# An attention stage woven into a matmul stage: other slots for the pieces from the fourteenth pair on, and another order of four small steps

## The reference

```python
# attention in chunks of 64 rows, per batch and head: q, k, v (8, 8, 576, 64)
scores = scale * q_c @ k_c.T ; scores -= max(scores) ; attn = exp(scores)
attn = attn / (sum(attn) + 1e-9) ; out = attn @ v_c
x = out as (4608, 512)
# first feed-forward, d_ff 1536
xn = x / sqrt(mean(x * x) + 1e-6) * rms_g
y = (silu(xn @ w_gate) * (xn @ w_val)) @ w_out
# second feed-forward, d_ff 2048
h = y @ w_in2 ; g = h * clip(h + 3, 0, 6) / 6 ; result = g @ w_out2
```

## Time and profile before

| | |
|---|---|
| median of 3 runs | 1655.23 us (1655.1 to 1658.37) |
| profiled execution, time | 1649.52 us |
| profiled execution, span | 1647.7 us |
| mean granted TensorE clock | 0.995 |
| PE busy | 1612.2 us (98%) |
| DVE, ACT, POOL busy | 1054.4, 859.0, 786.0 us |
| attention woven in | from about 45 us to about 357 us |

### The profile page before, as it was taken

How to read it: one execution, slowest core, us unless ns; L and a number is a source line. 1 busy time by engine, 2 the same in 40 slices (tenths; PEclk the granted TensorE clock), 3 DMA queues, 4 the chain that set the end, 5 groups by cost and what they waited for, 6 DMA issues and landing times.

```text
span 1647.7 us, 29730 instructions
## 1 busy us (share of the span) xinstructions
PE 1612.2 (98%) x11337; PEld 1572.1 (95%) x11337; DVE 1054.4 (64%) x1441; ACT 859.0 (52%) x1341; POOL 786.0 (48%) x772
## 2 busy tenths in 40 slices
PE   7889999999999999999999999999999999999998
PEld 5778898899999999999999999999999999999998
DVE  5877878868755555665555776656666865455454
ACT  4756666655544445554444565555655644434432
POOL 2543443449776665434240477777676631231231
PEclk9999999999999999999999999999999999999999
DMA  9677776644565655989997866556658986776674
GB/s 180 141 190 157 171 196 167 156 149 141 190 223 196 209 196 197 337 312 314 310 315 283 301 235 237 207 190 239 225 192 268 390 273 202 219 230 211 211 227 118
DMA packets 335646, 366.88 MB, mean 223 GB/s; under 512 B 186256, under 2 KB 299152, under 8 KB 332304
## 3 DMA queue, kind: packets, MB, share of 16 engines
q1 hardware_dynamic: 321584, 334.69, 64.1%
q0 software_dynamic: 8800, 28.85, 5.1%
q10 hardware_dynamic: 5120, 1.44, 0.5%
HBM read 200.80 MB, written 164.10 MB: 221 GB/s over the span
## 4 chain that ended last, share of the span: by engine, by line
PE 87%; DVE 3%; POOL 3%; issue 2%; SPq 2%; ACT 2%; DMA 1%; DVEq 0%; ACTq 0%; POOLq 0%
PE bx L968 14%; PE by L968 14%; PE bx L970 14%; PE bx L969 14%; PE by L970 14%; PE by L969 14%; SPq L568 1%; PE att L946 1%; DVE tx L1498 1%; PE att L895 1%; PE att L937 1%; DMA hl_b<-h_scratch 1%; PE att L918 1%; DVE wr L1511 1%; SPq L561 0%
## 5 line engine op out<-in xcount | busy, mean ns | idle before, releaser
L968 PE MATMUL bx<-tx,wr 128*128 128x384 f32 x840 | 288.0, 343 | 4.1 <-ACT gb L1176 2.0
L968 PE MATMUL by<-tx,wr 128*128 128x384 f32 x840 | 287.2, 342 | 0.1
L970 PE MATMUL bx<-tx,wr 128*128 128x384 f32 x840 | 281.9, 336 | 0.0
L969 PE MATMUL bx<-tx,wr 128*128 128x384 f32 x840 | 281.6, 335 | 0.0
L970 PE MATMUL by<-tx,wr 128*128 128x384 f32 x840 | 281.5, 335 | 0.0
L969 PE MATMUL by<-tx,wr 128*128 128x384 f32 x840 | 281.4, 335 | 0.0
L1549 DVE TENSOR_TENSOR hl_d<-hl_d 128x1536 fp32r<-128x1536 f32 x84 | 146.6, 1775 | 91.2 <-ACT hl_d L1248 91.2
L1867 POOL DMA_DIRECT2D out_dram<-ot x128 | 70.2, 556 | 248.3 <-DVE ot L1572 245.8
L1549 DVE TENSOR_TENSOR hl_b<-hl_b 128x1152 fp32r<-128x1152 f32 x84 | 117.9, 1419 | 105.5 <-ACT hl_b L1248 104.6
L1248 ACT ACTIVATE hl_d<-hl_d 128x1536 fp32r<-128x1536 f32 x84 | 123.3, 1486 | 112.5 <-DMA hl_d<-u_scratch 112.5
L968 PEld LDWEIGHTS bx<-tx,wr 128*128 128x128 f32 x840 | 158.2, 188 | 9.3 <-issue 3.1
(11 more groups left out here) (193 smaller groups left out, 3781.4 us busy)
## 6 DMA issues: line engine op xcount, KB each, us to landing
hl_d<-u_scratch SPq DMA_DIRECT2D x84, 768.0 KB, 4.5
hl_b<-h_scratch SPq DMA_DIRECT2D x84, 576.0 KB, 5.5
u_scratch<-ut SPq DMA_DIRECT2D x48, 576.0 KB, 3.7
h_scratch<-ht SPq DMA_DIRECT2D x36, 576.0 KB, 3.7
u_scratch<-ub SPq DMA_DIRECT2D x96, 192.0 KB, 2.8
u_scratch<-ub SPq DMA_DIRECT2D x48, 384.0 KB, 2.5
h_scratch<-vb SPq DMA_DIRECT2D x72, 192.0 KB, 3.3
h_scratch<-vb SPq DMA_DIRECT2D x36, 384.0 KB, 3.0
```

What stands on the lines that cost most here:

```text
L968: pe.matmul(dst, w_hi, m_hi, start=start, stop=False, skip_group_check=not opens)
L969: pe.matmul(dst, w_hi, m_lo, start=False, stop=False, skip_group_check=not opens)
L970: return pe.matmul(dst, w_lo, m_hi, start=False, stop=stop, skip_group_check=not opens)
```

## The change

For the pairs from 13 on, the slots of the four pieces are written anew. From pair 17 on AT of a pair lies in the slot of SC of the next pair (it was one slot behind it), and TensorE does AT first. XX lies five slots behind AT as before, and so in the slot of TR of the next pair, behind it. The pairs 13 to 17 lead over to that pattern. `AFTER` has new entries for when q and k of the next pair are transposed. The order of four steps within a slot changes too: ScalarE copies the probabilities ahead of the snapshots and of the mean square; VectorE scales the attention ahead of the maxima; GpSimd's inverse root comes at AT+2 in place of AT+3.

```diff
-    EARLY = {... 13: (38, 43, 48, 51), 14: (46, 49, 52, 58), 15: (51, 53, 59, 64), 16: (57, 61, 66, 73), 17: (64, 66, 75, 77)}
-    AFTER = {7: 5, 8: 1, 11: 5, 12: 5, 14: 1, 16: 5, 17: 5}
+    EARLY = {... 13: (40, 43, 46, 50), 14: (45, 49, 52, 57), 15: (51, 56, 59, 63), 16: (58, 62, 64, 68), 17: (63, 68, 70, 76)}
+    AFTER = {7: 5, 8: 1, 11: 5, 12: 5, 25: 5, 20: 1, 24: 1, 33: 1, 29: 5, 30: 1, 15: 5, 17: 3, 18: 3, 23: 5, 32: 5, 28: 3, 13: 3, 26: 3, 16: 3, 22: 1, 34: 1, 19: 5, 21: 5, 27: 3}
...
-        return EARLY[n][piece] if n in EARLY else 7 * n - 53 - min(3, (n - 12) // 2) + (0, 5, 8, 13)[piece]
+        return EARLY[n][piece] if n in EARLY else 7 * n - 53 - min(3, (n - 12) // 2) + (0, 5, 7, 12)[piece]
...  ScalarE, in each slot
+                n = woven(m, slot, TR, 1)
+                if n is not None:
+                    copy_probsT(n)
                 if slot in (1, 2):
                     snap_a(m, S1, slot - 1)
...
                 n = woven(m, slot, AT, 2)
                 if n is not None:
                     mean_square(n)
-                n = woven(m, slot, TR, 1)
-                if n is not None:
-                    copy_probsT(n)
...  VectorE, in each slot
+                n = woven(m, slot, AT, 1)
+                if n is not None:
+                    scale_attention(n)
                 n = woven(m, slot, SC, 1)
                 if n is not None and n + 1 < NN and next_transposed_after(n) == 1:
                     transpose_qk(n + 1)
                 if n is not None:
                     shift_scores(n)
-                n = woven(m, slot, AT, 1)
-                if n is not None:
-                    scale_attention(n)
...  GpSimd, in each slot
-                n = woven(m, slot, AT, 3)
+                n = woven(m, slot, AT, 2)
                 if n is not None:
                     inverse_rms(n)
```

More of the change, by code:

```diff
@@ L445, in chunked_attention_then_two_ffns @@
     S_FIRST = NG
-    EARLY = {6: (-6, -3, 1, 7), 7: (0, 3, 8, 12), 8: (7, 9, 14, 20), 9: (12, 15, 21, 24), 10: (18, 23, 26, 31), 11: (24, 28, 33, 37), 12: (32, 37, 39, 44), 13: (38, 43, 48, 51), 14: (46, 49, 52, 58), 15: (51, 53, 59, 64), 16: (57, 61, 66, 73), 17: (64, 66, 75, 77)}
-    AFTER = {7: 5, 8: 1, 11: 5, 12: 5, 14: 1, 16: 5, 17: 5}
+    EARLY = {6: (-6, -3, 1, 7), 7: (0, 3, 8, 12), 8: (7, 9, 14, 20), 9: (12, 15, 21, 24), 10: (18, 23, 26, 31), 11: (24, 28, 33, 37), 12: (32, 37, 39, 44), 13: (40, 43, 46, 50), 14: (45, 49, 52, 57), 15: (51, 56, 59, 63), 16: (58, 62, 64, 68), 17: (63, 68, 70, 76)}
+    AFTER = {7: 5, 8: 1, 11: 5, 12: 5, 25: 5, 20: 1, 24: 1, 33: 1, 29: 5, 30: 1, 15: 5, 17: 3, 18: 3, 23: 5, 32: 5, 28: 3, 13: 3, 26: 3, 16: 3, 22: 1, 34: 1, 19: 5, 21: 5, 27: 3}
     SC, TR, AT, XX = 0, 1, 2, 3
     def at_slot_of(n, piece):
-        return EARLY[n][piece] if n in EARLY else 7 * n - 53 - min(3, (n - 12) // 2) + (0, 5, 8, 13)[piece]
+        return EARLY[n][piece] if n in EARLY else 7 * n - 53 - min(3, (n - 12) // 2) + (0, 5, 7, 12)[piece]
     def next_transposed_after(n):
```

## The result

The changed kernel takes 1653.01 us (median of 22 runs, 1647.3 to 1658.86), the kernel before, run beside it, 1656.72 us (22 runs, 1653.98 to 1661.12). The ratio is 0.9981, with a 95% interval of 0.9972 to 0.999: 0.19% or 3.1 us faster (the two medians as they stand lie 3.7 us apart), just inside the 0.2% that I called no change. The forecast was 1652.8 us, 2.4 us faster. The profiled execution gives 1651.29 us with a span of 1649.5, which is 1.8 us *more* than the profiled one of before. A single profile of each can't give a change of 3 us, but its stretches can be compared one by one.

The account below looks back on a forecast made before the run. TensorE, 87% of the chain that ended last, was taken as the bound. Terms -3.6 + 0.1 + 0.6 + 1.2 - 0.2 - 0.5 = -2.4 us took 1655.2 to 1652.8 us; range 1649.3 to 1658 us.

Parts of the forecast that it names:

- A: TensorE's slots shared by attended rows and scores: each pair saves 0.20 us, 18 times, 3.6 us; bounds 0 and 3.8.
- B: First halves of steps: ScalarE's chain delays normed rows for the earlier x transposes, 0.1 us in six steps, +0.6 us.
- Rival 3: TensorE's shared slots: the pairing saves nothing, total 1656.4 us, no change to be told; chance 0.08.
- C: Steps with fills, VectorE the nearer bound: six half steps' gain of 0.20 us doesn't arrive, +1.2 us.
- D: Pairs 12 and 13: values wait stays, scores +0.83, pair 12's rows wait -1.7, pair 13 wait +0.7; sum -0.2 us.
- rival 2: Slots 5 and 12 of each step: x transposes come too soon and wait for normed rows; slower, chance 0.12.
- E: Pair 17's x transposes, now six slots behind attended rows in place of two: their wait goes, -0.5 us.
- Queues: Loads of values, q and k and stores of x shift slots; SyncE has time, all costed at nothing.
- number 1: Fill steps and first halves: VectorE's new order also removes the waits; sum -5.7 us, 1649.5 us; chance 0.38.

Follow-up runs that it names:

- e3: The changed kernel with attended rows and x transposes one slot later from pair 18 on, leaving one shared slot; 1656.39 us, 1.0013 of the kernel before.
- e5: The changed kernel with the two groups of a shared slot swapped, scores ahead of attended rows; 1653.90 us, 0.9982 of the kernel before.
- e7: The changed kernel with `AFTER` 5, 3, 3 in place of 3, 5, 1 for pairs 31, 32, 33; 1649.84 us, 0.9972 of the kernel before.
- e4: The changed kernel with GpSimd's inverse root back at its old slot, AT+3; 1652.29 us, 0.9979 of the kernel before.
- e2: The kernel before with the new orders and the earlier root alone, old slots and `AFTER`; 1655.35 us, 0.9999 of the kernel before.
- e8: The changed kernel with loads of q and k of pairs 14 and 15 issued from slot 30, not 26; 1652.83 us, 0.998 of the kernel before.
- e13: The changed kernel with the edits of e12, e7 and e8 together; 1644.87 us, 0.9944 of the kernel before.
- e1: The kernel before with the new slots and `AFTER` but all the old orders; 1673.73 us, 1.0114 of the kernel before.
- e10: The changed kernel with VectorE's old order alone, scaling the attention behind maxima and shift; 1672.77 us, 1.0097 of the kernel before.
- e12: The changed kernel with the new orders and early root only for pairs from 12 on; 1650.49 us, 0.9961 of the kernel before.

## Why the forecast came out

The size was near (3.1 us measured, 2.4 forecast), but that is in good part luck: a sum of terms that missed in both directions. The cause that I named, two groups in one slot, is shown by e3; the woven part, where my 2.4 us should have been, gained 5.9 in the profile (near 5 without the good fortune of step 6), and other places took some of it back.

**A, right in the mechanism, too small in size.** The step that failed was "I take 0.83 + 0.63 = 1.46 us for the two in place of 1.66". A pair costs 1.30 us, as the second group also starts 0.1 us sooner and not only saves its change of shape. 18 x 0.36 = 6.5 us for the forecast 3.6, beyond my bound of 3.8. e3 takes 17 of the pairs away and loses 3.5 us in the steps that hold them. That is less than 17 x 0.36 = 6.1, as e3 is also rid of the wait of B: its step 8 takes 19.7 us for 19.2, which is 2 x 0.36 less some 0.2; and in step 12 it is 0.5 us shorter than the changed kernel. e5 shows that the order of the two groups doesn't matter to it. Rival 3 is out.

**B, right, somewhat dearer.** A first half takes 9.70 us where the second takes 9.46: 0.24 us per half step, not 0.1; in step 10 it takes 9.97. In step 5 it is nothing (9.38), since pair 17's transposes still stand in slot 6 there, which I had overlooked. With steps 7, 8, 10, 11 and 13 that is 1.4 us, for 0.6. The rule of the Trainium skill, "ScalarE: Activation LUTs", section "What ACT_TABLE_LOAD costs", with its drain on top would have given 2.66 us between the start of the load and the exponentials; after the change it is 215.10 - 213.81 = 1.29 us, so there is none. (In the earlier trace rows it is 1.29 too, not the 1.31 that I wrote.)

**C, wrong but for step 12, and there worse than forecast.** I put the gain of six half steps (second halves of 5, 8 and 11, first halves of 6, 9 and 12) at nothing, since VectorE was "the nearer bound". The second halves of steps 8 and 11 take 9.46 us for 9.85, the full gain of a pair, and the first half of step 9 takes 10.40 for 10.64. The second halves of steps 6 and 9, of which I had said nothing, take 9.69 for 10.40 and 10.42. The step that failed is "The change takes nothing from its work": VectorE's busy time in the woven part fell from 227.86 to 219.82 us. 7.8 us of that are the same 38 fills, which took 51.4 us before and 43.6 after. Of the 2.1 us that a fill is busy in step 12, 0.94 are what it takes alone, and the rest is standing behind GpSimd's sum (see e7). Step 12 lost 1.8 us. e7 changes nothing but three slots at which q and k are transposed, and takes step 12 to 20.1 us; the wait in slot 0 goes as the fill there no longer stands behind a sum. Why the fills meet fewer sums after the change is not shown step by step.

**D, the part with the wrong reasons.** The wait for the values stayed (3.4 us for 2.8), as forecast. The clock's drop behind it is absent in the changed kernel's profile, but not because of the change. From slot 10 of step 2 to step 3 the granted clock is 1.00 there, and 0.71 to 0.85 in the mean in the kernel before and in all ten others that have this wait (e4: 0.71 over 11.9 us, e2: 0.84 over 10.9); only e8 and e13, without the wait, have 1.00 too (in e13 the clock falls 10 us later, in step 3). The changed kernel's profiled execution was a lucky one at this place: e2 and e4, with the same wait, take 10.90 and 11.87 us there for its 9.42, so the third line of the table above is no gain of the change. The wait of pair 12's rows is gone as forecast, but "with the root one slot sooner it runs ahead of that sum" is not the cause. It is gone in e1 (new slots, root late) and in e4 (new slots and orders, root late), so with the new slots the root wasn't needed. It is gone in e2 too, with the old slots, where orders and root changed together; which of the two does it there is not shown. Pair 13 waits 0.96 us where I put 0.7, in the eleven other kernels with the new slots 0.25 to 0.38. Whether its scores cost their 0.83 us I can't read: the wait that they once stood ahead of is 2.8 us before, 3.4 in e2, with them still ahead of it, and 2.1 to 3.8 in the kernels with the new slots.

**Orders at nothing: wrong, twice.** The sum has no term for the orders on VectorE and ScalarE. VectorE's is worth 20.8 us of the woven part (300.65 - 279.88): without it the sum of squares holds up the load of the table and the exponentials. My rival 2, "the normed rows are late because scores and scaling now ask for VectorE at the same time, and ScalarE's queue with its table load does the rest", describes what e1 and e10 do; the changed kernel escapes it by that one order. And the earlier root was not free: I wrote that the reader of the operand sum behind it "is a store". At pair 7 it is ScalarE's fill, and TensorE loses 0.9 us of the 1.1 in slot 6 of step 0 (2.18, with the late root 1.30, before 1.05). The rest of the 2.6 us in steps 0 to 2 is open: kernels with the new orders for all pairs took 70.9 to 73.7 us there, those with the old ones 68.7 and 68.9, but e12 and e13, which have the old ones up to pair 11, took 71.3 and 70.1.

**E**: pair 17's wait is gone, as forecast. **Step 15** has no term in my sum: the wait there (0.78 us, with its tail 1.05) is gone with the new slots. **Queues**: SyncE waits 35.9 us for attended rows in place of 45.5, and no wait of TensorE for a load is new.

Of the rivals, number 1 (the waits go as well) came true in steps 6 and 9 and was taken back in steps 0 to 2 and in step 12.

## What to carry to other kernels

When two pieces of work are put into one slot of one engine, ask first in which order *every other engine* gets to their results, and follow the piece at which an in-order queue (here ScalarE's sum of squares, then its table, then the exponentials) would stand: the pairing was worth 6.5 us of TensorE's time, and the wrong order behind it cost 20.8. A wait that ends last can hide a chain that is just as long, as e8 shows, where 3.5 us taken from one slot came back within the next step. Where pieces of uneven length share a queue, a small search over their slots, read in the profile step by step, is cheap: three numbers in a table gave 2.7 us in step 12 of one profile. And busy time is not always work: before an engine is called the bound, look whether the same instruction takes the same time everywhere.

## What the hardware showed that I had not expected

Two groups of 32 small matmuls (64 rows) back to back overlap at their border: the second group starts 0.52 us after the first, where a group alone holds the product back 0.63 us before it goes on and 0.83 in all. The same fill on VectorE (128 x 768) took 2.13 us in the changed kernel and 0.94 us in e7 a little sooner. What it stands behind is GpSimd: in 124 of 124 cases a fill that began well inside one of its sums ended 0.81 to 0.82 us after that sum, and where the fill began first (step 6 of the changed kernel) it took 0.93 and the sum 2.41 us, where in e7 it took 1.85.
